# A six-way butterfly split around the score weightings, and sequence tiles grouped by parity

## The chip, the cores and the metric

The kernel runs on one core of a Trainium2 chip. The metric is the device time of one execution in microseconds. Five engines have instruction streams of their own: TensorE (PE, with its weight loads as PEld), VectorE (DVE), ScalarE (ACT), GpSimd (POOL) and SyncE (SP), whose queue issues the loads and stores. They are tied together by semaphores alone: every stream runs in its written order and stops at each `wait_ge` until the counter has reached the value.

## The reference

Three stages follow each other. All is 32-bit float, with 2 batches, 768 positions and 512 features.

```python
# 1: attention with decay, 8 heads of 64, state carried from block to block
intra = (q_b @ k_b.T * Dmask) @ v_b
inter = (q_b * lam_pow) @ kv_state
kv_state = lam**block * kv_state + (k_b * rev_pow).T @ v_b
# 2: two-axis Fourier mixing, normalization, MLP 512 -> 2048 -> 512
mixed = real(fft(fft(x, axis=seq), axis=features))
u = x + mixed
un = (u - mean(u)) / sqrt(var(u) + 1e-6)
x2 = u + relu(un @ w_ch1) @ w_ch2
# 3: gate from a causal 5-tap convolution over positions
out = (sigmoid(conv(x2)) * (x2 @ w_val)) @ w_out
```

## The kernel before, in words

The sequence is cut into 12 chunks of 128 positions, n = 0 to 11; 0 to 5 are batch 0 and 6 to 11 batch 1. For every chunk, TensorE forms the scores (`scores`, line 408) in two PSUM banks, VectorE weights them with the decay into `probs` (`mask`, line 880), and TensorE multiplies them with the values (`from_chunk`, line 444) on top of what the state gives (`from_state`, line 433). The state is fed by `state_product` (line 420) and `fold_state` (lines 897 and 899), from decayed keys and queries that GpSimd prepares (`kd`, line 1174, and `qd`, line 1184). ScalarE copies each chunk's result to `xT` (`xT_copy`, line 685). TensorE's order in iteration n is scores(n+1), state_product(n), from_state(n), for n = 1 to 6 `hid_transform(n-1)`, from_chunk(n). As there is one set of score banks, scores(n+1) waits for mask(n).

The Fourier mixing runs beside this. `radix4(n)` on VectorE (lines 907 to 913) takes the first step over the features of one chunk, `hid_transform(n)` on TensorE (lines 464 to 466) the rest, and `spectrum_copy(n)` on ScalarE (lines 693 to 697, five copies counted in `s_ye`) puts the spectrum into `yy`, 128 x 514 values a chunk. Over the sequence axis the six chunks of a batch are first combined by a six-way butterfly on VectorE, 16 operations of 128 x 514, counted in `s_r6`:

- `chunk_pair(b, c)` for c = 0, 1, 2: sum and difference of chunks c and c + 3, into `sd` (lines 923 and 924). It needs the spectrum of chunk c + 3.
- `two_pairs(b)`: four operations on the first two pairs, into rows 0, 1, 3 and 4 of `yy` (lines 929 to 933).
- `third_pair(b)`: `chunk_pair(b, 2)` and six operations that add the third pair and complete rows 0 to 5 (lines 939 to 945).

For batch 0 the pieces stand in VectorE's loop over chunks at iterations 5, 6 and 7, each at the end of its iteration. There an iteration n runs `radix4(n-1)` (n = 1 to 6), `mask(n+1)`, `fold_state(n)` (but not at 5 and 11), then the pieces. At 8 and 9 it runs radix4(6) and radix4(7) last.

After the butterfly, ScalarE writes the mirrored half of the spectrum (`mirror`, line 705), and TensorE turns the rows into sequence outputs: `seq_tile(a)` for a = 0 to 3, six output groups g in two banks of three (lines 485, 486, 489). A group g = 0 or 3 takes two products, any other four. Groups 0, 2 and 4 read rows 0 to 2 of `yy`, groups 1, 3 and 5 rows 3 to 5. Tiles 0, 1 and 2 stand in TensorE's iteration 9, behind from_chunk(9), and tile 3 in iteration 10. `add_u(a)` on VectorE (line 954) adds each bank to `xT`. Then come the mean, the MLP in 32 steps of split-precision products, which fill TensorE to the end, and the gated projection. Batch 1 goes the same way, with its butterfly in the MLP steps 3, 4 and 5.

The order is written out by hand. The functions the diff touches, with what calls them:

Of the kernel before, what the change touches and what calls it, by code (L numbers as in the profile page):

```python
# [10 lines left out]
ALU = mybir.AluOpType  # L11
ACT = mybir.ActivationFunctionType

P = 128
# [41 lines left out]
def program(nc, qkv, lam, w_mlp, w_val, conv_w, w_out, seq_tab, hid_tab, out):  # L56
# [4 lines left out]
    NC = S // P  # L61
# [21 lines left out]
    with ExitStack() as ctx:  # L83
        def sem(name):
            return ctx.enter_context(nc.semaphore(name))

        def sb_in(stack, name, shape, dt=F32):
            return stack.enter_context(nc.sbuf_tensor(name, shape, dt))
# [57 lines left out]
        with ExitStack() as spectra:  # L146
            yy = sb_in(spectra, "yy", [P, B, NC, YW])
# [6 lines left out]
        with ExitStack() as fold:  # L154
            sd = sb_in(fold, "sd", [P, NC, YW])
        with ExitStack() as second_l:
# [21 lines left out]
        s_x, s_r4, s_hy, s_ye, s_r6, s_rev, s_f, s_u = (  # L178
            sem(n) for n in ("s_x", "s_r4", "s_hy", "s_ye", "s_r6", "s_rev", "s_f", "s_u"))
# [26 lines left out]
        def seq_part(g, i, n=P):  # L206
            at = SEQ_AT[g] + i * P
            return seq_c[:, at:at + n] if g < 4 else seq_up[:, at - LOW_TAB:at - LOW_TAB + n]


        R4, YE, R6 = 4, 5, 16

        def spec_bank(n):
            if n == NC + 1:
# [3 lines left out]
        def added_u(b, a, bank=1):  # L218

            return 2 * a + bank + 1 if b == 0 else 2 * R + 8 * a + 4 * (bank + 1)  # L220
# [69 lines left out]
        def spectrum(b, g, im, a):  # L290
            if a >= 2:
                return mirrored[:, g, im, (a - 2) * P:(a - 1) * P]
            return yy[:, b, g].rearrange("p (i k) -> p i k", i=2)[:, im, a * P:(a + 1) * P]
# [99 lines left out]
        def _(pe):  # L393
# [74 lines left out]
            def rows_of(g):  # L468

                return (4, 5) if g in (1, 5) else (1, 2)  # L470


            def seq_tile(a):
                if a == 0:
                    pe.wait_ge(s_r6, R6)
                    pe.wait_ge(s_seq, 32)
                if a == 2:
                    pe.wait_ge(s_rev, 4)
                for h, bank in ((0, ps[COS]), (1, ps[SIN])):
                    if a:  # L480
                        pe.wait_ge(s_u, added_u(0, a - 1, h))
                    for g in range(3 * h, 3 * h + 3):
                        o = bank[:, g % 3 * P:(g % 3 + 1) * P]
                        if g % 3 == 0:
                            mm(o, spectrum(0, g, 0, a), seq_part(g, 0), start=True, stop=False)
                            m = mm(o, spectrum(0, g, 1, a), seq_part(g, 1), start=False, stop=True)
                        else:
                            for i in range(4):
                                m = mm(o, spectrum(0, rows_of(g)[i % 2], i // 2, a),  # L489
                                       seq_part(g, i), start=i == 0, stop=i == 3)  # L490
                    m.then_inc(s_f, 1)
# [366 lines left out]
        def _(dve):  # L858
            tt = nc.vector.tensor_tensor
            stt = nc.vector.scalar_tensor_tensor  # L860
# [40 lines left out]
            def radix4(n):  # L901
                b, c = divmod(n, NC)
                x, z = xT[:, b, :, c * P:(c + 1) * P], zin[:, n % 2]
                dve.wait_ge(s_x, n + 1)
                if n > NC:
                    dve.wait_ge(s_r4, R4 * n)
                tt(esum[:, :, :], x[:, 0:2], x[:, 2:4], ALU.add).then_inc(s_r4, 1)
                if n >= 2:
                    dve.wait_ge(s_hy, n - 1)
                tt(z[:, 2:4], x[:, 0:2], x[:, 2:4], ALU.subtract).then_inc(s_r4, 1)  # L910
                dve.wait_ge(s_r4, R4 * n + 1)
                tt(z[:, 0], esum[:, 0], esum[:, 1], ALU.add).then_inc(s_r4, 1)
                tt(z[:, 1], esum[:, 0], esum[:, 1], ALU.subtract).then_inc(s_r4, 1)
# [4 lines left out]
            def chunk_pair(b, c):  # L918
                y = yy[:, b]
                dve.wait_ge(s_ye, YE * (b * NC + c + 4))  # L920
                if b == 0 and c == 0:
                    dve.wait_ge(s_set, 4)
                tt(sd[:, c], y[:, c], y[:, c + 3], ALU.add).then_inc(s_r6, 1)
                tt(sd[:, 3 + c], y[:, c], y[:, c + 3], ALU.subtract).then_inc(s_r6, 1)

            def two_pairs(b):
                y, at = yy[:, b], R6 * b
                dve.wait_ge(s_r6, at + 3)
                tt(y[:, 0], sd[:, 0], sd[:, 1], ALU.add).then_inc(s_r6, 1)
                dve.wait_ge(s_r6, at + 4)  # L930
                stt(y[:, 1], sd[:, 1], -0.5, sd[:, 0], ALU.mult, ALU.add).then_inc(s_r6, 1)
                tt(y[:, 3], sd[:, 3], sd[:, 4], ALU.subtract).then_inc(s_r6, 1)
                stt(y[:, 4], sd[:, 4], 0.5, sd[:, 3], ALU.mult, ALU.add).then_inc(s_r6, 1)

            def third_pair(b):
                y, at = yy[:, b], R6 * b
                chunk_pair(b, 2)
                dve.wait_ge(s_r6, at + 9)
                tt(y[:, 0], y[:, 0], sd[:, 2], ALU.add).then_inc(s_r6, 1)
                dve.wait_ge(s_r6, at + 10)  # L940
                tt(y[:, 2], sd[:, 1], sd[:, 2], ALU.subtract).then_inc(s_r6, 1)
                tt(y[:, 5], sd[:, 4], sd[:, 5], ALU.add).then_inc(s_r6, 1)
                stt(y[:, 1], sd[:, 2], -0.5, y[:, 1], ALU.mult, ALU.add).then_inc(s_r6, 1)
                tt(y[:, 3], y[:, 3], sd[:, 5], ALU.add).then_inc(s_r6, 1)
                stt(y[:, 4], sd[:, 5], -0.5, y[:, 4], ALU.mult, ALU.add).then_inc(s_r6, 1)


            def add_u(a):
                ug = u[0][:, a].rearrange("p (c g) -> p g c", g=NC)
                xg = xT[:, 0, a].rearrange("p (c g) -> p g c", g=NC)  # L950
                for h, bank in ((0, ps[COS]), (1, ps[SIN])):
                    three = slice(3 * h, 3 * h + 3)
                    dve.wait_ge(s_f, 2 * a + h + 1)
                    tt(ug[:, three], bank[:, 0:3 * P].rearrange("p (g c) -> p g c", g=3), xg[:, three],
                       ALU.add).then_inc(s_u, 1)
# [81 lines left out]
            for n in range(N):  # L1037
                if 1 <= n <= NC:
                    radix4(n - 1)
                if n + 1 < N:  # L1040
                    mask(n + 1)
                if n % NC < NC - 1:
                    fold_state(n)
                if n == NC - 1:
                    chunk_pair(0, 0)
                if n == NC:
                    chunk_pair(0, 1)
                    two_pairs(0)
                if n == NC + 1:
                    third_pair(0)  # L1050
                if n in (8, 9):
                    radix4(n - 2)
                if n == N - 3:
                    for a in range(R - 1):
                        add_u(a)
# [44 lines left out]
            def mlp_step(st, after):  # L1100
                if after:
                    hidden_lo(after)
                if st.m == M - 1:
                    finish_mlp(2, nc.vector, dve)
                if st.last:
                    add_mlp(st)
                for n in RADIX_AT.get(st.m, ()):
                    radix4(n)
                if st.m == 3:
                    chunk_pair(1, 0)  # L1110
                if st.m == 4:
                    chunk_pair(1, 1)
                    two_pairs(1)
                if st.m == 5:
                    third_pair(1)
                    add_eps(0)
                    add_eps(1)
                if 6 <= st.m < 6 + R:
                    add_pair(st.m - 6)
                if st.m == 9:  # L1120
                    hidden_sum(1, 3, nc.vector, dve)
                if st.m == 11:
                    centre(1, 0)
                    centre(1, 1)
                if st.m in (12, 13):
                    cen_lo(1, st.m - 12)
                if st.m == 17:
                    add_eps(2)
                    add_eps(3)
                if st.m in (18, 19):  # L1130
                    newton(st.m - 18)
                if st.m in (19, 20):
                    finish_mlp(st.m - 19, nc.vector, dve)
                if st.m in (21, 22):
                    x3_lo(st.m - 21)
                if 22 <= st.m < 22 + TAPS:
                    two, d = divmod(st.m - 22, K - 1)
                    taps(0, 2 * two, d + 1)
# [138 lines left out]
```

## Time and profile before

| | |
|---|---|
| median of 3 runs | 458.53 us (458.24 to 458.71) |
| the profiled execution | 459.72 us, its span 457.9 us |
| mean granted TensorE clock | 0.988 |
| PE busy | 438.7 us (96%) |
| PEld busy | 420.1 us (92%) |
| DVE busy | 268.2 us (59%) |
| ACT busy | 151.9 us (33%) |
| POOL busy | 147.0 us (32%) |

Busy times are sums over an engine's instructions within the span. The chunks 0 to 9 take the first 69 us of the span; the MLP begins at about 97 us. In a timeline row the first number is the start in us from the span's start, the second the time from the first instruction's start to the last one's end (several instructions of a kind are merged, xN). The ends overlap the next start by some 0.1 us, so the time that an operation takes in a stream is read from start to start. In brackets stands the engine's idle time before the row and what ended it.

### The profile page before, as it was taken

The page shows a single profiled execution, that of the slowest core. Times are in us where ns is not written, and L with a number is a line of the kernel's source. Part 1 is how long each engine was busy: PE and PEld are TensorE (multiplying, and loading weights), DVE is VectorE, ACT ScalarE, POOL GpSimd, SP SyncE. Part 2 cuts the span into 40 slices and gives each one's busy share as a digit, 9 for nine tenths or more (in the row PEclk, how much of TensorE's full clock was granted, in tenths as well). Part 3 has the DMA queues.
Part 4 walks back from the last instruction along what each step waited for, and adds up shares of the span by engine and source line. Part 5 has one row for each costly group of instructions (what it writes and reads, how often), then busy time and mean ns, then how long its engine had stood idle before and what let it go on. Part 6 is the DMA issues. An engine that isn't in the chain of part 4 may idle for free.

```text
span 457.9 us, 7070 instructions
## 1 busy us (share of the span) xinstructions
PE 438.7 (96%) x2892; PEld 420.1 (92%) x2892; DVE 268.2 (59%) x419; ACT 151.9 (33%) x284; POOL 147.0 (32%) x99
## 2 busy tenths in 40 slices
PE   6799859999999999999999999999999999999997
PEld 5688749989999999999999999999999999889985
DVE  1657993566835974643533424966565557999220
ACT  1154343065322141111524217344125134525312
POOL 1432536235523222332376422332422450600000
PEclk9899979999999999999999999999999999999999
DMA  6977810050220220202022022022022020001112
GB/s 209 320 219 269 289 67 2 1 183 20 73 94 0 93 77 16 92 1 94 1 93 92 1 92 94 0 93 92 1 92 93 0 93 2 0 1 70 69 47 92
DMA packets 14032, 37.05 MB, mean 81 GB/s; under 512 B 1576, under 2 KB 3120, under 8 KB 14000
## 3 DMA queue, kind: packets, MB, share of 16 engines
q1 hardware_dynamic: 14000, 36.60, 23.8%
q8 instruction: 23, 0.38, 0.3%
q14 instruction: 9, 0.07, 0.0%
HBM read 33.44 MB, written 3.15 MB: 80 GB/s over the span
## 4 chain that ended last, share of the span: by engine, by line
PE 87%; DVE 7%; DMA 3%; ACT 1%; issue 1%; SPq 1%; DVEq 0%
PE ps L550 10%; PE ps L552 9%; PE ps L573 9%; PE ps L572 9%; PE ps L571 9%; PE ps L551 9%; PE ps L489 3%; PE ps L657 2%; PE ps L656 2%; PE ps L655 2%; PE ps L433 2%; PE ps L408 2%; PE ps L634 2%; PE ps L635 2%; PE ps L636 2%; PE ps L444 2%
## 5 line engine op out<-in xcount | busy, mean ns | idle before, releaser
L741 ACT ACTIVATE hh<-ps 128x384 fp32r<-128x384 f32 x64 | 31.5, 492 | 173.1 <-PE ps L552 173.1
L1017 DVE SCALAR_TENSOR_TENSOR hl<-ps,hh 128x384 fp32r<-128x384 f32 x64 | 35.3, 556 | 83.3 <-ACT hh L741 83.3
L550 PE MATMUL ps<-cen_h,w1h_a 128*128 128x384 f32 x128 | 44.1, 344 | 0.5 <-DVE hl L1017 0.5
L550 PE MATMUL ps<-cen_h,w1h_b 128*128 128x384 f32 x128 | 44.2, 345 | 0.0
L552 PE MATMUL ps<-cen_h,w1l_b 128*128 128x384 f32 x128 | 43.1, 337 | 0.0
L552 PE MATMUL ps<-cen_h,w1l_a 128*128 128x384 f32 x128 | 43.1, 337 | 0.0
L573 PE MATMUL ps<-hh,w2l_b 128*128 128x384 f32 x128 | 43.1, 337 | 0.0
L572 PE MATMUL ps<-hl,w2h_b 128*128 128x384 f32 x128 | 43.1, 337 | 0.0
L571 PE MATMUL ps<-hh,w2h_b 128*128 128x384 f32 x128 | 43.1, 337 | 0.0
L551 PE MATMUL ps<-cen_l,w1h_a 128*128 128x384 f32 x128 | 43.1, 337 | 0.0
L551 PE MATMUL ps<-cen_l,w1h_b 128*128 128x384 f32 x128 | 43.0, 336 | 0.0
L571 PE MATMUL ps<-hh,w2h_a 128*128 128x384 f32 x128 | 42.9, 335 | 0.0
L572 PE MATMUL ps<-hl,w2h_a 128*128 128x384 f32 x128 | 42.9, 335 | 0.0
L573 PE MATMUL ps<-hh,w2l_a 128*128 128x384 f32 x128 | 42.9, 335 | 0.0
L1034 DVE TENSOR_TENSOR xT<-xT,ps 128x384 f32<-128x384 f32 x56 | 30.6, 553 | 17.8 <-PE ps L573 17.7
L1075 DVE SCALAR_TENSOR_TENSOR xT<-u_pad,cw,xT 128x768 f32<-128x768 f32 x32 | 37.9, 1246 | 0.0
L1189 POOL TENSOR_TENSOR w1l_b<-raw_b,w1h_b 128x1024 fp32r<-128x1024 f32 x8 | 19.9, 2492 | 47.9 <-ACT w1h_b L710 47.9
L1189 POOL TENSOR_TENSOR w2l_a<-raw_a,w2h_a 128x1024 fp32r<-128x1024 f32 x8 | 19.2, 2399 | 47.4 <-ACT w2h_a L710 47.4
L1189 POOL TENSOR_TENSOR w2l_b<-raw_b,w2h_b 128x1024 fp32r<-128x1024 f32 x8 | 19.3, 2412 | 43.9 <-ACT w2h_b L710 43.9
L1189 POOL TENSOR_TENSOR w1l_a<-raw_a,w1h_a 128x1024 fp32r<-128x1024 f32 x8 | 21.1, 2640 | 28.9 <-ACT w1h_a L710 28.9
L408 PE MATMUL ps<-chunks 64*128 64x128 f32 x192 | 15.8, 310 | 13.0 <-DVE probs L880 11.5
L408 PEld LDWEIGHTS ps<-chunks 64*128 64x128 f32 x192 | 13.4, 210 | 15.1 <-issue 13.1
(179 smaller groups left out, 1045.5 us busy)
## 6 DMA issues: line engine op xcount, KB each, us to landing
raw_a<-in_mlp SPq DMA_DIRECT2D x16, 512.0 KB, 4.8
raw_b<-in_mlp SPq DMA_DIRECT2D x16, 512.0 KB, 4.4
chunks<-in_qkv SPq DMA_DIRECT2D x12, 512.0 KB, 5.5
chunks<-in_qkv SPq DMA_DIRECT2D x22, 256.0 KB, 4.9
out<-out_sb SPq DMA_DIRECT2D x12, 256.0 KB, 2.0
raw_a<-in_val SPq DMA_DIRECT2D x2, 512.0 KB, 4.5
raw_b<-in_out SPq DMA_DIRECT2D x2, 512.0 KB, 4.6
seq_c<-const_seq SPq DMA_DIRECT2D x1, 768.0 KB, 5.8
```

Of the source, the lines that this page charges most:

```text
L408: m = mm(ps[SCORE[par]][:, hp * P:(hp + 1) * P], kT[c][rows, hp, :], qT[c][rows, hp, :], start=True, stop=True)
L550: mm(bank, wh_, xh, start=r == 0, stop=False)
L551: mm(bank, wh_, xl, start=False, stop=False)
L552: m = mm(bank, wl_, xh, start=False, stop=r == R - 1)
L571: mm(bank, w2h[st.slot][:, j, r], hh[:, slot, j], start=st.first and j == 0, stop=False)
L572: mm(bank, w2h[st.slot][:, j, r], hl[:, slot, j], start=False, stop=False)
L573: m = mm(bank, w2l[st.slot][:, j, r], hh[:, slot, j], start=False, stop=st.last and j == 1)
L741: nc.scalar.activation(hh[:, slot, j], ps[j][:, 0:TB], ACT.Relu).then_inc(s_hh, 1)
L1017: stt(hl[:, slot, j], ps[j][:, 0:TB], 0.0, hh[:, slot, j].bitcast(F32), ALU.max, ALU.subtract).then_inc(s_hl, 1)
L1034: tt(acc[:, r], acc[:, r], ps[4 + r][:, 0:TB], ALU.add).then_inc(s_add, 1)
L1075: stt(xT[:, b, r], u_pad[b][:, r, PAD - d:PAD - d + S], cw[:, K - 1 - d, r:r + 1], xT[:, b, r], ALU.mult, ALU.add).then_inc(s_tap, 1)
L1189: tt(lo, r_, hi.bitcast(F32), ALU.subtract).then_inc(s_wl, 1)
```

## The change

The butterfly of either batch is cut anew. `third_pair` becomes `third_even`, which makes the third pair and completes rows 0, 2 and 1, and `third_odd`, which completes rows 3, 5 and 4. In batch 0, `chunk_pair(0, 1)` and `two_pairs(0)` go from iteration 6 to iteration 5, `third_even(0)` stands in iteration 6 and `third_odd(0)` in iteration 7. Batch 1 runs both in the place of `third_pair(1)`. A sequence tile puts the even groups in the first bank and the odd ones in the second, and tile 0 waits for the 13 signals that complete the even rows before the first bank and for all 16 before the second; `add_u` follows in its slices.

```diff
-        R4, YE, R6 = 4, 5, 16
+        R4, YE, R6, R6_EVEN = 4, 5, 16, 13
...
             def seq_tile(a):
                 if a == 0:
-                    pe.wait_ge(s_r6, R6)
                     pe.wait_ge(s_seq, 32)
...
                 for h, bank in ((0, ps[COS]), (1, ps[SIN])):
+                    if a == 0:
+                        pe.wait_ge(s_r6, R6 if h else R6_EVEN)
                     if a:
                         pe.wait_ge(s_u, added_u(0, a - 1, h))
-                    for g in range(3 * h, 3 * h + 3):
-                        o = bank[:, g % 3 * P:(g % 3 + 1) * P]
+                    for g in range(h, NC, 2):
+                        o = bank[:, g // 2 * P:(g // 2 + 1) * P]
...
-            def third_pair(b):
+            def third_even(b):
                 y, at = yy[:, b], R6 * b
                 chunk_pair(b, 2)
-                dve.wait_ge(s_r6, at + 9)
+                dve.wait_ge(s_r6, at + 10)
                 tt(y[:, 0], y[:, 0], sd[:, 2], ALU.add).then_inc(s_r6, 1)
-                dve.wait_ge(s_r6, at + 10)
                 tt(y[:, 2], sd[:, 1], sd[:, 2], ALU.subtract).then_inc(s_r6, 1)
+                stt(y[:, 1], sd[:, 2], -0.5, y[:, 1], ALU.mult, ALU.add).then_inc(s_r6, 1)
+
+            def third_odd(b):
+                y = yy[:, b]
+                tt(y[:, 3], y[:, 3], sd[:, 5], ALU.add).then_inc(s_r6, 1)
                 tt(y[:, 5], sd[:, 4], sd[:, 5], ALU.add).then_inc(s_r6, 1)
-                stt(y[:, 1], sd[:, 2], -0.5, y[:, 1], ALU.mult, ALU.add).then_inc(s_r6, 1)
-                tt(y[:, 3], y[:, 3], sd[:, 5], ALU.add).then_inc(s_r6, 1)
                 stt(y[:, 4], sd[:, 5], -0.5, y[:, 4], ALU.mult, ALU.add).then_inc(s_r6, 1)
...
-                    three = slice(3 * h, 3 * h + 3)
+                    three = slice(h, NC, 2)
...
                 if n == NC - 1:
                     chunk_pair(0, 0)
-                if n == NC:
                     chunk_pair(0, 1)
                     two_pairs(0)
+                if n == NC:
+                    third_even(0)
                 if n == NC + 1:
-                    third_pair(0)
+                    third_odd(0)
...
                 if st.m == 5:
-                    third_pair(1)
+                    third_even(1)
+                    third_odd(1)
```

## Rows read from the trace of the kernel before

**Rows 1.** The page, granted TensorE clock in 40 slices of 11.4 us, in tenths

```profile
PEclk9899979999999999999999999999999999999999
```

**Rows 2.** Waits, 40 to 70 us: us in total, times, longest

```profile
PE ps L408 <- DVE probs L880: 6.6, 2, 5.0
```

**Rows 3.** Chain of waits, 30 to 100 us: start, us, what ran

```profile
61.28 1.30 DVE probs L880 x2
...
62.72 2.08 PE ps L408 x16
64.80 1.05 PE ps L420 x16
65.85 1.96 PE ps L433 x8
...
68.83 0.42 PE ps L485 x2
```

**Rows 4.** Windows: stretch, us and its busy us of PE, clock, DMA share, GB/s

```profile
57.70:60.80 3.10, 0.00 (x1) 1.00 0.50 181
...
62.70:67.60 4.90, 4.88 (x40) 0.50 0.01 3
```

**Rows 5.** Timeline of ScalarE, 42 to 48 us

```profile
43.30 0.51 ACT L697 COPY yy<-ps 128x256 f32<-128x256 f32 x1
...
47.41 0.29 ACT L693 COPY yy<-ps 128x64 f32<-128x64 f32 x1 [2.93 <-PE ps L466]
...
47.85 0.51 ACT L697 COPY yy<-ps 128x256 f32<-128x256 f32 x1
```

**Rows 6.** Timeline of VectorE, 42 to 64 us

```profile
44.51 0.43 DVE L907 TENSOR_TENSOR esum<-xT 128x256 f32<-128x256 f32 x1 [0.86 <-ACT xT L685]
...
52.37 1.29 DVE L880 TENSOR_TENSOR probs<-ps,decay 128x512 f32<-128x512 f32 x2
...
54.48 0.70 DVE L923 TENSOR_TENSOR sd<-yy 128x514 f32<-128x514 f32 x1
...
55.69 0.69 DVE L939 TENSOR_TENSOR yy<-yy,sd 128x514 f32<-128x514 f32 x1
56.30 1.55 DVE L941 TENSOR_TENSOR yy<-sd 128x514 f32<-128x514 f32 x1
57.77 1.67 DVE L942 TENSOR_TENSOR yy<-sd 128x514 f32<-128x514 f32 x1
59.36 0.68 DVE L943 SCALAR_TENSOR_TENSOR yy<-sd,yy 128x514 f32<-128x514 f32 x1
...
60.56 0.68 DVE L945 SCALAR_TENSOR_TENSOR yy<-sd,yy 128x514 f32<-128x514 f32 x1
```

**Rows 7.** Timeline of GpSimd, 42 to 70 us

```profile
45.71 1.06 POOL L1174 TENSOR_TENSOR kd<-chunks,decay 128x512 f32<-128x512 f32 x1 [6.81 <-PE ps L420]
...
55.74 1.55 POOL L1174 TENSOR_TENSOR kd<-chunks,decay 128x512 f32<-128x512 f32 x1 [2.37 <-PE ps L420]
```

**Rows 8.** Timeline of TensorE's products, 42 to 64 us

```profile
44.87 0.69 PE L420 MATMUL ps<-chunks,kd 128*64 128x64 f32 x16
45.83 0.68 PE L464 MATMUL ps<-hid_c,zin 128*128 128x128 f32 x4 [0.27 <-DVE zin L913]
...
47.30 1.09 PE L444 MATMUL ps<-probs,chunks 128*64 128x128 f32 x16
...
53.81 1.16 PE L408 MATMUL ps<-chunks 64*128 64x128 f32 x16 [1.59 <-DVE probs L880]
...
56.61 1.09 PE L444 MATMUL ps<-probs,chunks 128*64 128x128 f32 x16
```

**Rows 9.** Timeline of ScalarE, 60 to 66 us

```profile
61.28 3.05 ACT L705 ACTIVATE sd<-yy 128x768 f32<-128x768 f32 x4 [2.95 <-DVE yy L945]
64.24 1.26 ACT L679 ACTIVATE state_l<-state,rstd 128x128 f32<-128x128 f32 x4
```

**Rows 10.** Timeline of SyncE's queue, 40 to 100 us

```profile
50.14 2.44 SPq L328 DMA_DIRECT2D chunks<-in_qkv  x3
```

## The prediction

> **What bounds the kernel now.** I read the page's busy times first (the table above): TensorE works for 96% of the span and VectorE for 59%, so anything that helps must let TensorE wait less, or run at its higher clock more. The line of the granted clock in the slices shows one deep dent, in the sixth slice, which covers 57 to 69 us [rows 1]. The waits of the stretch 40 to 70 us name the reason: twice the score products of line 408 waited for VectorE's score weighting `mask` (line 880), 6.6 us together, and once for 5.0 us [rows 2]. The chain of waits shows the second price: after `mask(9)` ended, scores, state product, state read and chunk product (lines 408, 420, 433, 444) took from 62.72 to 68.83 us, and then the sequence transform of batch 0 began [rows 3]. The windows say that the clock was 1.00 up to 60.8 us, by then TensorE had stood still for 3 us, and 0.50 (1.2 GHz of 2.4) while it worked again until 67.6 us [rows 4]. From 68.83 us on TensorE has work back to back up to batch 0's mean, so what the change does to the time is what it does to the start of `seq_tile(0)`.
>
> **What moves.** The butterfly's 16 operations (128x514) stay 16. Before, VectorE runs two of them behind `mask(6)`, six behind `mask(7)`, and eight, `third_pair`, between `mask(8)` and `mask(9)`; after, it is eight, five and three. Two groups move: `chunk_pair(0,1)` and `two_pairs`, six operations, from behind `mask(7)` to before `radix4(5)` and `mask(7)`; and five of `third_pair`'s eight from behind `mask(8)` to before it. None crosses a DMA of its own; the loads that follow late products are priced below.
>
> **Step 1, the middle part.** It needs chunk 4's spectrum: the last copy starts at 43.30 us and lasts 0.51 us, 43.81 us [rows 5]. VectorE is free by then (it next starts at 44.51 us, and its idle time before that is 0.86 us) [rows 6], so the six operations begin at 43.84 us. One takes 0.60 us to the next one's start (from 59.36 to 60.56 us there are two), six 3.60 us. But GpSimd asks for its `kd` at 45.71 us and for `qd` right behind it [rows 7], both tied to products that the change leaves in place. The trace shows what this costs: with `kd` of 55.74 us beside it, line 941 took 1.47 us to the next start instead of 0.60, and line 942, beside the `qd` that follows, 1.59 us [rows 6, 7]: 0.87 and 0.99 more. Line 939, which had started 0.05 us before the request, was not held (55.69 us); the next one was. Sum: 43.84 + 3.60 + 1.86 = 49.30 us. The bounds are no hold at all (47.44 us) and both held as in those rows; I take the second, since the operations and requests are of the same kinds.
>
> The Trainium skill, SBUF — State Buffer, section "Who interferes with whom", states that a VectorE instruction with two SBUF inputs and a GpSimd instruction that reads SBUF exclude each other for the whole instruction, whoever issues first going first. By the page each held operation would lose up to GpSimd's whole unhindered length, 1.06 and 1.18 us, hence 49.68 us; the rows above, 0.87 and 0.99 us, agree with it in kind and decide the size. It speaks against this change, because it is this move that brings the six operations under those two requests.
>
> **Step 2, who waits.** Queued behind on VectorE: `radix4(5)`, `mask(7)`, `fold_state(6)`. `radix4(5)` starts at 49.30 us instead of 44.51 us. `hid_transform(5)` started 1.32 us after it (45.83 us) [rows 6, 8], now 50.62 us. TensorE has done its state product at 44.87 + 0.69 = 45.56 us, so it stands still for 5.06 us, where it waited 0.27 us; behind it queue the chunk product of 6, the scores of 8 and all the rest. `mask(7)` follows right behind `radix4`, so from about 50.5 us for its 1.29 us [rows 6], over 2 us before TensorE comes to the scores of 8 that want it.
>
> **Step 3, the clock.** A standstill of 5.01 us ended in a half clock [rows 3, 4, 8]; this one is as long, so I expect the same. Scores, state product and state read took 5.09 us at the low clock (2.08, 1.05, 1.96) [rows 3] against 2.80 us at the high one (53.81 to 56.61 us) [rows 8], 1.82 times. `hid_transform(5)` streams 1.47 us (45.83 to 47.30 us) [rows 8], so it loses 1.2 us: its copies start not 1.58 us after it (47.41 - 45.83) but 2.78 us, at 53.40 us, take 0.95 us (47.41 to 47.85 + 0.51) [rows 5], and chunk 5's spectrum is there at 54.35 us. The bounds are 0 (no fall) and 1.5 us.
>
> **Step 4, the even part.** Five operations from 54.40 us. Starts at 0, 0.60, then 1.32 (the new wait for the difference of its own pair adds about 0.1 us), 1.92, 2.52 us; `mask(8)` follows the last by 0.72 us (60.56 to 61.28 us) [rows 3, 6]: 57.64 us. GpSimd's `kd(8)` is asked for when the state product of 7 ends: chunk product 6 from 53.3 us, 1.02 us at the high clock and up to 0.8 us more at the low one, scores 1.09 us, product 0.69 us, request 0.15 us later (45.56 to 45.71 us), that is 56.25 to 57.05 us. The last two operations start at 56.32 and 56.92 us. I take one held operation, 0.87 us, so `mask(8)` starts at 58.51 us; none gives 57.64 us, two give 59.50 us. Before it started at 52.37 us.
>
> **Step 5, the odd part.** From `mask` to the operation behind it are 2.11 us (52.37 to 54.48 us), from `mask` to the scores behind it 1.44 us (52.37 to 53.81 us). The scores of 9 thus start at 59.95 us and the three odd operations at 60.62, 61.22 and 61.82 us. `kd(9)` is asked for 3.37 us after `mask(8)` started (52.37 to 55.74 us) [rows 6, 7], at 61.88 us, 0.06 us after the last of the three has started: not held. `mask(9)` starts 0.72 us behind it, at 62.54 us, the scores of 10 at 63.98 us. A hold there (by 0.06 us it is a near thing) costs 0.87 us. TensorE has finished chunk product 8 at 59.95 + 2.80 + 1.02 = 63.77 us, so it idles 0.2 us where it idled 5.01 us.
>
> **Step 6, the gain given back.** With no standstill the clock stays high: 2.80 + 1.02 = 3.82 us instead of 6.11 us to the sequence transform, which starts at 67.80 us instead of 68.83 us. So 1.26 us lost at the scores of 10 and 2.29 us won by the clock: 1.03 us gained.
>
> **What is hidden or free.** The parity grouping leaves ten products in either bank (one two-product and two four-product tiles each), and `add_u` still reads 384 dense PSUM columns; its writes keep their inner stride and change only the outer one: nothing, with bounds of 0.1 us per call either way, and hidden, since `add_u` waits for TensorE's banks. What stands before the first `add_u` comes later, however: `mirror` on ScalarE follows the copy of chunk product 8 (64.4 us) and takes 3.05 us, the state decay 1.26 us [rows 9], then VectorE's fold 0.9 us and `radix4(7)` 1.2 us, so that `add_u` can start at 70.8 us and end at 71.7 us; TensorE wants it at 67.80 + 4.46 = 72.3 us. The cover is 0.6 us, and beyond it each microsecond costs one. The release of the even part (13 signals instead of 16) is worth nothing: TensorE reaches it 3 us after all 16 are out. The load of chunk 10's keys and queries, issued at 50.14 us [rows 10], moves with chunk product 6 to about 56.2 us, lands about 5 us later, and is wanted at 63.98 us: cover 2.8 us, beyond which each microsecond costs one. Batch 1's same two functions run back to back in the MLP, where VectorE waits anyway; 0.1 us there is hidden.
>
> **The rivals.**
> (a) Two operations held instead of one, in the even part, or one there and one in the odd: 0.87 to 0.99 us back, gain about 0.1 us, 458.4 us. For it: the margins of 0.06 us. Against: the low clock pushes `kd(8)` late.
> (b) No hold in the even part, because TensorE recovers its clock later: gain 1.6 to 1.9 us, 456.8 us. After 62.72 us the low clock lasted 4.9 us [rows 4], which from 50.62 us would reach 55.5 us.
> (c) The clock stays high through the new standstill: 1.2 us earlier from step 3, of which a further hold eats 0.99 us at worst; gain 1.2 to 2.2 us, 456.8 us. Against: [rows 4].
> (d) GpSimd doesn't hold the moved operations: `radix4(5)` at 47.44 us, a standstill of 3.2 us, everything 1.9 to 3.1 us earlier up to the scores of 9 and then bounded by TensorE: seq_tile(0) near 64 us, gain near 5 us, 453.6 us. Against: [rows 6, 7].
> (e) Slower: one mechanism, the half clock in exchange. In the median runs the old standstill may not have brought the clock down (they are 1.19 us under the profiled one), while the new one does. Then the start was 68.83 - 2.29 = 66.54 us and becomes 67.80 us: 1.26 us slower, 459.8 us. It decides once the old low-clock stretch costs under 1.26 us in the timed runs.
>
> **How the numbers follow.** The profiled execution took 459.72 us, 457.9 us of it span; 459.72 - 1.03 = 458.69 us. The median of the runs is 458.53 us, 1.19 us below, and I take the gain off that: 457.5 us. Chances: the forecast with its one held operation 0.43 (own spread 0.5 to 1.6 us of gain), (a) 0.21, (b) 0.15, (c) 0.09, (d) 0.02, (e) 0.10. The range, 455.9 to 459.2 us, leaves out (d), the fast end of (b) and (c), and most of (e). What can be told from no change is about 0.2%, 0.92 us. Faster: somewhat over half of the forecast's, nearly all of (b), (c) and (d), 0.49. Same: the rest of the forecast and (a), 0.39. Slower: (e) and a bit of (a), 0.12.
>
> **What would show it.** In the profile after: `radix4(5)` at 49.3 us with two held operations ahead of it (steps 1, 2); no line-408 wait of 5 us, but a wait of about 5 us of line 464 for line 913 and the clock at 0.50 right behind it (step 3); one long operation among the even five, none among the odd three (steps 4, 5); lines 408 to 444 of chunk 9 in 3.8 us at clock 1.00, and the first sequence product at 67.8 us (step 6). It is wrong if the standstill before `hid_transform(5)` is far from 5 us, if `mask(8)` starts before 57 or after 59.5 us, or if the tail behind the first sequence product changes its length by over 0.3 us.

## The result, and the profile after

The changed kernel takes 463.01 us (median of 4 runs, 462.54 to 463.44) against 458.62 us for the kernel before: ratio 1.0092, 95% interval 1.0072 to 1.0112. It is slower by 4.4 us, outside the range of the prediction and on the other side of its forecast of 457.5 us. The profiled execution took 463.44 us with a span of 461.6 us.

The page's clock line (slices of 11.5 us, in tenths) now has deep dents in its fifth and seventh slice, 46 to 58 us and 69 to 81 us, where [rows 1] had one in its sixth. The dent in the second slice stands in both and lies before anything that the change moves.

```profile
PEclk9799798999999999999999999999999999999999
```

The waits from 38 to 120 us (who waited for whom; us in total, times, longest) have no line 408 waiting for `mask` any more; [rows 2] is gone. Two others stand there, and one on VectorE:

```profile
PE ps L464 <- DVE zin L915: 5.1, 1, 5.1
PE ps L487 <- DVE u_pad L958: 3.7, 1, 3.7
...
DVE state L899 <- ACT state_l L681: 2.1, 1, 2.1
```

The first was forecast. The second was not: TensorE stands at the first product of the second sequence tile and waits for `add_u(0)`. The timeline from 38 to 76 us, with the product of the mean behind it, shows how it comes about (start, us; in brackets the idle time before; most rows left out). This trace runs 0.60 us ahead of that of before up to the change (the scores of 6 start at 38.63 us against 39.23 us).

```profile
48.72 0.41 DVE L909 TENSOR_TENSOR esum<-xT 128x256 f32<-128x256 f32 x1
50.02 1.19 PE L464 MATMUL ps<-hid_c,zin 128*128 128x128 f32 x4 [5.06 <-DVE zin L915]
52.85 1.98 PE L444 MATMUL ps<-probs,chunks 128*64 128x128 f32 x16
...
53.90 0.69 DVE L925 TENSOR_TENSOR sd<-yy 128x514 f32<-128x514 f32 x1 [2.04 <-ACT yy L699]
...
57.17 1.29 DVE L882 TENSOR_TENSOR probs<-ps,decay 128x512 f32<-128x512 f32 x2
57.30 1.06 POOL L1180 TENSOR_TENSOR kd<-chunks,decay 128x512 f32<-128x512 f32 x1 [9.06 <-PE ps L420]
...
59.19 1.16 PE L408 MATMUL ps<-chunks 64*128 64x128 f32 x16
...
60.59 0.68 DVE L949 SCALAR_TENSOR_TENSOR yy<-sd,yy 128x514 f32<-128x514 f32 x1
...
61.30 1.29 DVE L882 TENSOR_TENSOR probs<-ps,decay 128x512 f32<-128x512 f32 x2
...
63.01 1.16 PE L408 MATMUL ps<-chunks 64*128 64x128 f32 x16
...
63.61 3.06 ACT L707 ACTIVATE sd<-yy 128x768 f32<-128x768 f32 x4
...
66.56 1.26 ACT L681 ACTIVATE state_l<-state,rstd 128x128 f32<-128x128 f32 x4
66.83 0.49 PE L487 MATMUL ps<-seq_c,yy 128*128 128x128 f32 x2
...
67.96 0.88 DVE L899 TENSOR_TENSOR state<-ps,state_l 64x256 f32<-64x256 f32 x2 [2.07 <-ACT state_l L681]
...
69.32 2.52 POOL L1195 TENSOR_TENSOR w1l_a<-raw_a,w1h_a 128x1024 fp32r<-128x1024 f32 x1 [2.17 <-ACT w1h_a L712]
69.54 2.45 DVE L914 TENSOR_TENSOR zin<-esum 128x128 f32<-128x128 f32 x1
...
71.80 2.39 POOL L1195 TENSOR_TENSOR w2l_a<-raw_a,w2h_a 128x1024 fp32r<-128x1024 f32 x1
71.91 2.42 DVE L915 TENSOR_TENSOR zin<-esum 128x128 f32<-128x128 f32 x1
...
74.37 1.60 DVE L958 TENSOR_TENSOR u_pad<-ps,xT 128x384 f32<-128x384 f32 x2
75.27 0.49 PE L487 MATMUL ps<-seq_c,yy 128*128 128x128 f32 x2 [3.71 <-DVE u_pad L958]
...
96.42 1.56 PE L521 MATMUL ps<-out_sb,ones 128*128 128x384 f32 x4
```

The same two places in the trace of before, the first sequence product and the product of the mean:

```profile
68.76 0.49 PE L485 MATMUL ps<-seq_c,yy 128*128 128x128 f32 x2
...
92.76 1.56 PE L519 MATMUL ps<-out_sb,ones 128*128 128x384 f32 x4
```

The upper half is the prediction's own schedule. The first sequence product starts at 66.83 us, in this trace's time 1.33 us earlier than before (68.76 - 0.60 - 66.83). The lower half is the loss. Two operations of `radix4(7)`, lines 914 and 915, take 2.45 and 2.42 us; unhindered each takes 0.28 us (`radix4(7)` below, in the version whose split waits). Beside each runs one of GpSimd's first two weight splits (line 1195, 2.52 and 2.39 us). `add_u(0)` is queued behind them and starts at 74.37 us, though its products were ready from about 69.4 us (in the versions below whose `add_u(0)` waits for nothing else, it starts 2.54 us after the first sequence product). TensorE stands still for 3.71 us, and then works at the low clock for a while, as the windows show (us, busy us of PE, clock):

```profile
71.60:75.20 3.60, 0.00 (x0) 1.00 0.00 0
75.20:80.00 4.80, 4.73 (x27) 0.64 0.00 0
```

The books close. From the first sequence product to the product of the mean TensorE needed 24.00 us before (68.76 to 92.76 us) and needs 29.59 us now (66.83 to 96.42 us), 5.59 us more. Of these 3.71 us are the standstill, and 1.72 us are the low clock: the second tile takes 6.19 us (75.27 to 81.46 us) where it took 4.47 us (73.33 to 77.80 us), and the later tiles are as long as before. The remaining 0.16 us lie around the standstill itself. Less the 1.33 us and the 0.60 us of the earlier start that is 3.66 us, and the spans differ by 3.7 us. Behind the product of the mean all traces of this document are equally long, 365.1 to 365.3 us.

### The profile page after: what moved, and what is told of

The parts are those of the page before. It is cut to its first block, busy times and chain, and to the rows that moved or that the text cites. A ratio compares the mean times of both kernels' runs of the same rounds, so it can differ in the third digit from the quotient of the medians.

```text
span 461.6 us, 7070 instructions
## 1 busy us (share of the span) xinstructions
PE 441.4 (96%) x2892; PEld 422.2 (91%) x2892; DVE 270.3 (59%) x419; ACT 151.5 (33%) x284; POOL 146.1 (32%) x99
## 4 chain that ended last, share of the span: by engine, by line
PE 86%; DVE 7%; DMA 3%; ACT 2%; issue 1%; SPq 1%; DVEq 0%
PE ps L552 9%; PE ps L554 9%; PE ps L574 9%; PE ps L575 9%; PE ps L553 9%; PE ps L573 9%; PE ps L491 3%; PE ps L659 2%; PE ps L658 2%; PE ps L657 2%; PE ps L444 2%; PE ps L433 2%; PE ps L408 2%; PE ps L636 2%; PE ps L637 2%; PE ps L638 2%
## 5 line engine op out<-in xcount | busy, mean ns | idle before, releaser
L1195 POOL TENSOR_TENSOR w2l_a<-raw_a,w2h_a 128x1024 fp32r<-128x1024 f32 x8 | 19.2, 2404 | 47.4 <-ACT w2h_a L712 47.4
L552 PEld LDWEIGHTS ps<-cen_h,w1h_a 128*128 128x128 f32 x128 | 24.1, 188 | 1.3 <-issue 0.7
L553 PEld LDWEIGHTS ps<-cen_l,w1h_b 128*128 128x128 f32 x128 | 24.2, 189 | 0.3
```

What stands on the lines that cost most here:

```text
L552: mm(bank, wh_, xh, start=r == 0, stop=False)
L553: mm(bank, wh_, xl, start=False, stop=False)
L1195: tt(lo, r_, hi.bitcast(F32), ALU.subtract).then_inc(s_wl, 1)
```

## The experiments

Theory H: the butterfly's move itself wins about a microsecond, and loses 5.6 us because `fold_state(9)` and with it `radix4(7)` now come late enough to meet the weight splits on GpSimd, which hold them. The fold is late since the state decay of chunk 9 stands on ScalarE behind `mirror(0)`, which now starts 2.3 us after `mask(9)` and not with it (it is queued behind the copy of chunk 8, which starts at 63.12 us now and started at 57.75 us before the change). Rival P: the parity grouping costs. Rival C: the standstill before `hid_transform(5)` and its low clock cost.

**Each part alone.** The parity grouping on the old order:

```diff
-                    for g in range(3 * h, 3 * h + 3):
-                        o = bank[:, g % 3 * P:(g % 3 + 1) * P]
+                    for g in range(h, NC, 2):
+                        o = bank[:, g // 2 * P:(g // 2 + 1) * P]
...
-                    three = slice(3 * h, 3 * h + 3)
+                    three = slice(h, NC, 2)
```

> The kernel before with the parity grouping of sequence tiles and of add_u alone; the order on VectorE is the old one. Theory H (the two last operations of radix4(7) meet GpSimd's 2.4 us weight splits, and TensorE waits for the add_u behind them): nothing in the order changed, so 458.6 us within 0.5, and each add_u 0.85 us as before. Rival P (the regrouped banks or the strided slices cost): 460 to 463 us, with add_u or the sequence products longer.

Measured: 459.13 us (10 runs) against 459.16 us, ratio 1.0009 (0.9986 to 1.0032). These runs spread from 457.04 to 462.48 us, so the interval is wide and would hide a cost of up to 1.5 us, but the profile has the waits of before, and an `add_u` of the same length:

```profile
70.51 0.87 DVE L954 TENSOR_TENSOR u_pad<-ps,xT 128x384 f32<-128x384 f32 x1 [1.84 <-PE ps L489]
```

And the order alone, without the grouping (the reverse of the diff above, and all 16 signals awaited once):

> The changed kernel with the old grouping of the sequence tiles (0 to 2 and 3 to 5) and one wait for all 16 signals; only the butterfly's order is new. Theory H: 463.0 us within 0.5, with the same wait of 3.7 us of the second sequence tile for add_u(0). Rival P: back to 458 us or below.

Measured: 465.11 us (4 runs, 462.80 to 469.48), ratio 1.0149 (1.0102 to 1.0196). The median is 2.1 us above the expected 463.0 us, but the wait is there without the grouping, to 0.01 us (3.72 and 3.71 us); rival P falls. The profiled execution was the slowest of the four and has one more wait, of line 408:

```profile
PE ps L487 <- DVE u_pad L958: 3.7, 1, 3.7
PE ps L408 <- DVE probs L882: 2.7, 1, 2.7
```

In this execution TensorE was back at its full clock for the chunk product of 6 (1.10 us, where it took 1.98 us in the changed kernel's trace). `kd(8)` was asked for 1.90 us after the even part's start and not 3.40 us, and two even operations were held:

```profile
55.88 0.69 DVE L925 TENSOR_TENSOR sd<-yy 128x514 f32<-128x514 f32 x1 [2.04 <-ACT yy L699]
...
57.78 1.06 POOL L1180 TENSOR_TENSOR kd<-chunks,decay 128x512 f32<-128x512 f32 x1 [7.55 <-PE ps L420]
57.82 1.57 DVE L942 TENSOR_TENSOR yy<-sd 128x514 f32<-128x514 f32 x1
...
59.31 1.67 DVE L943 SCALAR_TENSOR_TENSOR yy<-sd,yy 128x514 f32<-128x514 f32 x1
```

So the same order can come out either way, by when the clock recovers. That this is also what spreads the timed runs is not shown.

**Three ways out of the hold.** Each takes another piece of the chain away and leaves the butterfly's order. First, `mirror(0)` on ScalarE behind the copy of chunk 9:

```diff
-                if n == 8:
-                    mirror(0)
                 if n == 9:
+                    mirror(0)
                     split_group(0, 0)
```

> The changed kernel with mirror(0) on ScalarE moved behind the copy of chunk 9, ahead of the weight group's copies; the state decay of chunk 9 then no longer stands behind 3 us of mirror. Theory H: fold_state(9) starts about 2 us earlier (66 us), radix4(7) ends before GpSimd's splits, which themselves come 3 us later; the wait of 3.7 us and the low clock after it (5.6 us together) go: 457.4 us, 1.2 below the kernel before. Rival C (what costs is the standstill of 5 us before hid_transform(5) and its low clock): 462 to 463 us, as these stay.

Measured: 457.99 us (12 runs), ratio 0.9984 (0.9968 to 1.0001). In its timeline the fold comes at 65.91 us, `radix4(7)` from 66.80 to 68.15 us, `add_u(0)` waits 1.20 us for TensorE, not the reverse, and the split comes at 71.47 us:

```profile
65.91 0.86 DVE L898 TENSOR_TENSOR state<-ps,state_l 64x256 f32<-64x256 f32 x2
...
69.35 0.86 DVE L957 TENSOR_TENSOR u_pad<-ps,xT 128x384 f32<-128x384 f32 x1 [1.20 <-PE ps L491]
...
71.47 2.38 POOL L1194 TENSOR_TENSOR w1l_a<-raw_a,w1h_a 128x1024 fp32r<-128x1024 f32 x1 [4.34 <-ACT w1h_a L712]
```

The 5 us wait of line 464 is still there, so rival C falls too as the cause of this loss. This removes two things at once, the late fold and the early split. The next two keep the late fold and differ in the split. In the second, GpSimd's first split waits for `add_u(0)`:

```diff
                 if n == 10:
+                    pool.wait_ge(s_u, 2)
                     split_group(0, 0)
```

> The changed kernel with one more wait on GpSimd: its first weight splits wait for add_u(0) (two signals of s_u). mirror and fold_state(9) stay where they are. Theory H: fold_state(9) still waits 2 us for the state decay, but radix4(7) takes 1.2 us instead of 5.5, add_u(0) starts at 70.1 us, the wait of the second tile is 0 and the time 457.4 us within 0.6. Were it not the hold but the late fold_state(9) that counts, the time would stay near 463 us.

Measured: 458.51 us (10 runs), ratio 0.9994 (0.9968 to 1.0020). `radix4(7)` starts as late as in the changed kernel, at 69.06 us, and is through in 1.16 us:

```profile
69.06 0.43 DVE L909 TENSOR_TENSOR esum<-xT 128x256 f32<-128x256 f32 x1
...
69.74 0.28 DVE L914 TENSOR_TENSOR zin<-esum 128x128 f32<-128x128 f32 x1
69.94 0.28 DVE L915 TENSOR_TENSOR zin<-esum 128x128 f32<-128x128 f32 x1
...
70.26 0.86 DVE L958 TENSOR_TENSOR u_pad<-ps,xT 128x384 f32<-128x384 f32 x1
```

In the third, ScalarE and GpSimd stay as they are and `radix4(7)` goes ahead of the fold that it was queued behind:

```diff
+                if n == 9:
+                    radix4(7)
                 if n % NC < NC - 1:
                     fold_state(n)
...
-                if n in (8, 9):
-                    radix4(n - 2)
+                if n == 8:
+                    radix4(6)
```

> The changed kernel with radix4(7) ahead of fold_state(9) on VectorE (it needs nothing of it), mirror and the splits where they are. Theory H: radix4(7) runs at about 65.9 to 67.1 us, before GpSimd's first split; fold_state(9) still waits for the state decay until 68 us and ends at 68.9 us, add_u(0) starts with its products at 69.1 us: no wait of the second tile, 457.6 us within 0.6, as with the two other ways out. Were the late fold itself the cause, the time would stay near 463 us.

Measured: 457.75 us (10 runs), ratio 0.9989 (0.9965 to 1.0014). The fold starts at 68.12 us, later than in the changed kernel, the split at 69.13 us, earlier, and it does no harm, since beside it VectorE has only `add_u` to run, which reads PSUM and is 0.88 us long:

```profile
68.12 0.87 DVE L899 TENSOR_TENSOR state<-ps,state_l 64x256 f32<-64x256 f32 x2
...
69.13 2.37 POOL L1197 TENSOR_TENSOR w1l_a<-raw_a,w1h_a 128x1024 fp32r<-128x1024 f32 x1 [1.95 <-ACT w1h_a L712]
...
69.39 0.88 DVE L958 TENSOR_TENSOR u_pad<-ps,xT 128x384 f32<-128x384 f32 x1 [0.40 <-PE ps L491]
```

So it is neither the late fold alone nor the split alone, but the split beside `radix4(7)`. The control, the kernel before with the same late mirror:

> The kernel before with mirror(0) behind the copy of chunk 9 and nothing else. Theory H: there radix4(7) already ended before the first weight split and no tile waited, so the late mirror wins nothing: the same as the kernel before within 0.3 us. Rival: the late mirror helps by itself (by its place on ScalarE), then 457 to 458 us, and the gain of the changed kernel with a late mirror belongs to it.

Measured: 458.82 us (12 runs) against 459.06 us, ratio 0.9995 (0.9983 to 1.0007): the late mirror wins nothing by itself. Its profiled execution took 457.66 us, 1.2 us less than the median, and still has the standstill of 5.01 us and the low clock behind it:

```profile
61.19 2.08 PE L408 MATMUL ps<-chunks 64*128 64x128 f32 x16 [5.01 <-DVE probs L879]
```

**The middle part alone.** `third_even(0)` and `third_odd(0)` together where `third_pair(0)` was:

```diff
-                if n == NC:
-                    third_even(0)
                 if n == NC + 1:
+                    third_even(0)
                     third_odd(0)
```

> The changed kernel with third_even(0) and third_odd(0) together behind mask(8), where third_pair(0) was: only the middle part is moved. Both the 5 us standstill before hid_transform(5) and a long one before the scores of 10 are then there. mask(8) starts with the end of the scores of 8 at 55.9 us, mask(9) about 8.3 us later at 64.5 us, the scores of 10 at 66 us: 1.5 to 4 us behind the kernel before, 460 to 462.5 us. mirror starts together with mask(9) again, so the late fold and the held radix4(7) are not expected; were they tied to the middle part alone, 465 us.

Measured: 464.37 us (4 runs), ratio 1.0116 (1.0086 to 1.0145). The direction is as expected, and the size lies 1.9 us above the expected range: more operations were held than I had counted (four, lines 925, 942, 943 and 912), and both standstills are there, with no wait of the second tile. Waits of TensorE:

```profile
PE ps L464 <- DVE zin L915: 5.1, 1, 5.1
PE ps L408 <- DVE probs L882: 4.6, 1, 4.6
```

Thus the middle part in chunk 5 is a loss of its own, of about 5 us, which moving the even part as well buys back: the three versions above have medians of 457.75 to 458.51 us.

**The clock in the 5 us standstill.** On the version with the late mirror, TensorE is kept at work ahead of `hid_transform(5)`:

```diff
+                if n == 5:
+                    for _ in range(19):
+                        mm(ps[SPEC][:, 0:P], ones[:, :], ones[:, :], start=True, stop=True)
                 pe.wait_ge(s_r4, R4 * (n + 1))
```

> The version with the late mirror, and 19 more products of ones into the spectrum bank in TensorE's standstill before hid_transform(5) (their results are overwritten). Theory: the standstill costs through the clock; with it filled, hid_transform(5) streams in 1.47 instead of 2.83 us and the following products of chunk 6 and the scores of 8 run at clock 1.00. Without further holds the sequence transform begins 1.4 us earlier, with one or two held operations in third_even 0 to 0.5 us: 456.0 to 457.8 us against the 458.0 of the same without them. Rival: the clock isn't what delays the even part: no difference.

Measured: 459.12 us (12 runs), ratio 1.0004 (0.9990 to 1.0019); a miss, its median 1.1 us above the version without, with intervals that overlap. Its timeline:

```profile
44.05 4.51 PE L462 MATMUL ps<-ones 128*128 128x128 f32 x38
...
53.56 1.06 POOL L1182 TENSOR_TENSOR kd<-chunks,decay 128x512 f32<-128x512 f32 x1 [6.14 <-PE ps L420]
53.62 1.55 DVE L944 TENSOR_TENSOR yy<-sd 128x514 f32<-128x514 f32 x1
...
55.09 1.67 DVE L945 SCALAR_TENSOR_TENSOR yy<-sd,yy 128x514 f32<-128x514 f32 x1
...
58.23 2.08 PE L408 MATMUL ps<-chunks 64*128 64x128 f32 x16 [2.71 <-DVE probs L884]
```

The filling works as meant, and the even part begins 1.4 us sooner behind `radix4(5)` (3.78 us after it instead of 5.18 us). But with TensorE fast, `kd(8)` is asked for 1.89 us after the even part's start and no longer 3.19 us: two operations are held, 0.87 and 0.99 us, TensorE waits 2.71 us for `mask(8)`, and its clock falls there. The low clock at `hid_transform(5)` had kept GpSimd's request out of the even part. This was rival (a) with (c), and I had priced it as a gain.

**Versions that use what was found.** In the first the old middle part stays, and only the third pair's own two operations stand between `mask(8)` and `mask(9)`. The six others come behind `mask(9)`, where TensorE has 3.8 us of products ahead of the first tile and needs the odd rows only for its second bank. It also has the late mirror, GpSimd's splits behind `add_u(2)` and the parity grouping. Against the kernel before (`third_even` no longer makes the pair):

```diff
                 if n == NC + 1:
-                    third_pair(0)
+                    chunk_pair(0, 2)
+                if n == NC + 2:
+                    third_even(0)
+                    third_odd(0)
...
+                if n == 9:
+                    add_u(0, (0,))
+                    radix4(6)
+                    add_u(0, (1,))
+                    radix4(7)
+                    mask(10)
+                    add_u(1, (0,))
+                    fold_state(9)
+                    add_u(1, (1,))
+                    add_u(2)
+                    continue
```

> The order of the kernel before up to the first five operations of third_pair's place, but only the pair's own two operations stand between mask(8) and mask(9); the six others follow fold_state(8), even rows first; then the two halves of add_u, radix4(6), radix4(7), mask(10) and fold_state(9) interleaved; parity grouping, mirror behind the copy of chunk 9, the first weight splits on GpSimd behind add_u(2). Theory H with the counts of the prediction (held operations 0.9 us, a clock that falls only after a long standstill): mask(9) starts at 55.7 instead of 61.3 us, no standstill over 2 us, the first sequence product at 61.5 us, 7.3 us before that of the kernel before; 451.5 us within 1. Rival C (work of VectorE is only shifted and the tail waits for it instead): the add_u halves come late and half or more comes back, 455 us or more.

Measured: 453.25 us (4 runs) against 458.98 us, ratio 0.9873 (0.9852 to 0.9894), faster than either kernel by far more than the spread. The first sequence product starts at 61.13 us, and of the standstills 1.6 and 0.6 us are left; the clock has no dent there:

```profile
55.49 1.29 DVE L880 TENSOR_TENSOR probs<-ps,decay 128x512 f32<-128x512 f32 x2
...
61.13 0.49 PE L486 MATMUL ps<-seq_c,yy 128*128 128x128 f32 x2
```

The first sequence product comes where it was expected (7.3 us earlier than before, in the trace's own time), but the whole is 1.8 us short of the expected 451.5 us. From there to the product of the mean TensorE needs 25.02 us instead of 24.00 us, with 0.6 us of wait for the odd rows, of which GpSimd held all three operations. Which of the accompanying changes this version needs was not tried one by one.

The attempt to take away the 1.6 us as well, with `two_pairs` behind `mask(8)` and the third pair behind `mask(9)`:

```diff
                 if n == NC:
                     chunk_pair(0, 1)
+                if n == NC + 1:
                     two_pairs(0)
-                if n == NC + 1:
-                    chunk_pair(0, 2)
                 if n == NC + 2:
+                    chunk_pair(0, 2)
```

> The version with six operations behind mask(9), with two_pairs also moved, from behind mask(7) to behind mask(8), and the third pair's own two operations behind mask(9). The standstill of 1.6 us before the scores of 9 goes; mask(9) then ends no later than TensorE's products of chunk 8 by my count, but the even rows are complete only at 60.5 to 62 us, since VectorE has the same work up to there. Expected 452.5 to 453.5 us, so at most 0.7 us better than that version; if the held operations fall badly 454 us.

Measured: 456.38 us (6 runs), ratio 0.9939 (0.9916 to 0.9962): a miss, better than both kernels, 3.1 us worse than the other version. The wait before the scores of 9 is gone, but one of 1.12 us for `mask(9)` stands before the scores of 10. All three even operations are held, so TensorE waits 2.98 us for the even rows, and its clock falls about 1 us after it has begun the tiles (0.63 of the full clock from 64 to 66 us, 0.52 from 66 to 68 us):

```profile
58.55 1.54 DVE L938 TENSOR_TENSOR yy<-yy,sd 128x514 f32<-128x514 f32 x1
...
60.02 1.67 DVE L939 TENSOR_TENSOR yy<-sd 128x514 f32<-128x514 f32 x1
61.61 1.67 DVE L940 SCALAR_TENSOR_TENSOR yy<-sd,yy 128x514 f32<-128x514 f32 x1
```

## Why the prediction was wrong

Point by point, with the prediction's times less the 0.60 us by which this trace runs ahead:

- **Step 1** right: `radix4(5)` forecast at 48.70 us, found at 48.72 us, with two held operations ahead of it.
- **Steps 2 and 3** right: standstill 5.06 us as forecast, `hid_transform(5)` at 50.02 us as forecast, low clock behind it, even part at 53.90 us against 53.80 us.
- **Step 4** wrong by one held operation: the low clock lasted until about 56 us, so the scores of 8, counted at 1.09 us, took 1.71 us to the state product, and `kd(8)` was asked for at 57.30 us, after the even part was over. `mask(8)` started at 57.17 us, forecast 57.91 us and 57.04 us with none. That is rival (b). In the six traces with this order none of the five was held in four and two were held in the other two; the one hold of the forecast never came.
- **Step 5** right in kind: no long operation among the odd three, no long wait of line 408. But the delayed TensorE came to the scores of 9 at 59.19 us, so what was won at `mask(8)` was mostly not used.
- **Step 6** right: chunk 9's products in 3.82 us, the first sequence product at 66.83 us against 67.20 us. Up to here the forecast was too cautious by 0.3 us (1.33 us gained, 1.03 forecast).
- **What is hidden or free** is the step that failed: it put the hold of `radix4(7)` at nothing. It named the right chain (copy of chunk 8, `mirror`, state decay, fold, `radix4(7)`, first `add_u`) and gave it a cover of 0.6 us, with `radix4(7)` at its unhindered 1.2 us. The fold came even sooner than counted (67.96 us against 68.1 us). What I left out is GpSimd's queue at that place: the weight splits, which follow the copies of the weight group behind chunk 9's copy, are there from 69.3 us, and the last two operations of `radix4(7)` read two operands from SBUF. I had applied the holds of [rows 6, 7] to the operations that the diff moves, not to those that the move makes late. With this term, 4.3 us for two holds (2.45 + 2.42 - 0.56), `add_u(0)` is at 74.4 us, 3.7 us too late for TensorE, and the low clock and the restart add 1.9 us: the gain of 1.3 us becomes a loss of 4.3 us. The medians differ by 4.4 us; the profiled executions differ by 3.7 us, as the later one had its 0.60 us from before the change.

Rival (e) had named the direction, slower, but not this way: it needed the old low-clock stretch to cost under 1.26 us in the timed runs. From the scores of 10 to the first sequence product the three traces of the old order (the kernel before, the parity grouping alone, the late mirror alone) take 6.04, 5.67 and 5.47 us against 3.82 us at the full clock. The low clock thus cost 2.2, 1.9 and 1.6 us, and the last of the three is the run of 457.66 us.

The Trainium skill, SBUF — State Buffer, "Who interferes with whom", was quoted in the prediction for holds of a length set by GpSimd's instruction. Here the trace agrees by its letter: the two operations of 0.28 us last as long as the splits beside them, 2.45 us beside 2.52 us and 2.42 us beside 2.39 us. By that rule the split, and not `kd`, was the dangerous neighbour.

The tail behind the first sequence product, which the prediction named as something that would refute it if it changed by over 0.3 us, changed by 5.59 us, all of it ahead of the product of the mean.

What stays open: the three versions without the hold have medians 0.7 to 1.2 us under the runs of the kernel before beside them, but the interval of each includes 1. Their traces point the same way: from the scores of 7 to the product of the mean they take 47.3 to 47.4 us, and the three traces of the old order 48.4 to 49.0 us, one trace for each version. That the changed order is faster than the kernel before once the hold is gone is therefore likely, and not shown.

## What to carry to other kernels

Work moved off one wait makes whatever is queued behind it late; follow that chain to the next instruction that another engine needs, and at each operation on it ask what the engines that can hold it run at that time, not only at the operations that moved. An operation of 0.3 us with two SBUF operands can cost as much as the longest GpSimd instruction near it. The largest gain here, 5.7 us, came with moving work behind the last `mask` that TensorE waits for, to where TensorE has products enough of its own, and not in front of an earlier one.

## What the runs showed that I had not expected

TensorE's clock fell after a standstill much shorter than 5 us. In the version with the filled standstill it waited 2.71 us, and the scores behind it took 2.08 us instead of 1.16 us, at a granted clock of 0.50 (1.2 GHz); the order alone, with the same wait of 2.71 us, shows the same. In the version with `two_pairs` behind `mask(8)` it fell behind a wait of 2.98 us. A wait of 1.6 us before the scores of 9 left it at 1.00, in the kernel before as in the fastest one. After the 3.71 us of the changed kernel it fell only when TensorE was at work again, at about 76.5 us, and came back at about 80 us.

A low clock can help. It made TensorE's state product late, and with it GpSimd's request, so that VectorE's even part ran unheld. With the full clock the traces show two held operations, both in the version with the filled standstill and in the order alone; the former's median was 1.1 us higher, within overlapping intervals.
